# Attention, soft mixture and feed-forward in one kernel: ScalarE's order at the end of a round, and the second head's results in the other half of the partitions

## The reference

```python
def _attn_ref(r, k, v, w, u):            # B 4, H 8, S 768, D 48
    state = zeros(B, H, D, D)
    for t in range(S):
        kt, vt, rt, wt = k[:, :, t], v[:, :, t], r[:, :, t], w[:, :, t]
        cur = einsum('bhd,bhe->bhde', u[None] * kt, vt)
        y[:, :, t] = einsum('bhd,bhde->bhe', rt, state + cur)
        state = wt[..., None] * state + einsum('bhd,bhe->bhde', kt, vt)
    return y
# x = y as (B*S, H*D) = 3072 x 384, then
# _moe_ref: soft mixture with 8 experts of 4 slots, x @ phi, two softmaxes, relu MLPs of 1024
# _moe2_ref: h = relu(x @ w_in) (3072 x 2048); (h * h) @ w_out
```

## Time and profile before

| what | us |
|---|---|
| median of 3 runs | 537.76 |
| lowest and highest run | 533.3, 538.28 |
| the profiled execution | 541.06 |
| its span | 539.1 |
| of it, from the span's start to the end of attention's last copy | 252.1 |
| a round in the middle (level(rd, 0, 1) to the next) | 26.6 |

### The profile page before, as it was taken

One profiled execution on the slowest core, in us unless ns is written; L12 is line 12 of the kernel. 1 busy time (PEld: TensorE's weight loads), 2 busy tenths in 40 slices (PEclk: granted clock), 3 DMA queues, 4 the chain that ended last, 5 costly groups with the idle time before them and its releaser, 6 DMA issues.

```text
span 539.1 us, 18119 instructions
## 1 busy us (share of the span) xinstructions
PE 487.9 (91%) x7516; PEld 432.1 (80%) x7516; DVE 334.0 (62%) x583; ACT 333.9 (62%) x689; POOL 13.7 (3%) x21
## 2 busy tenths in 40 slices
PE   5688989798989898788889899999999999999996
PEld 3576878687878786777435489999999999999996
DVE  8687888788888787743441286555555555555552
ACT  5677786778787777453222376666566656665663
POOL 9000000000000000000000000000000000000000
PEclk9888999999999999979999999999999999999999
DMA  8785375757363614764999430101010101010101
GB/s 166 135 171 117 69 180 110 179 114 127 60 125 64 119 26 139 212 208 136 316 399 373 144 117 1 45 1 45 0 46 1 44 0 44 0 44 1 45 0 44
DMA packets 129385, 56.19 MB, mean 104 GB/s; under 512 B 103328, under 2 KB 128928, under 8 KB 128928
## 3 DMA queue, kind: packets, MB, share of 16 engines
q1 hardware_dynamic: 126112, 54.53, 38.6%
q10 hardware_dynamic: 3200, 0.59, 0.6%
HBM read 50.38 MB, written 4.72 MB: 102 GB/s over the span
## 4 chain that ended last, share of the span: by engine, by line
PE 71%; ACT 11%; SPq 6%; issue 5%; DVE 4%; DMA 2%; ACTq 0%; DVEq 0%
PE bank L758 13%; PE bank L760 12%; PE bank L759 12%; PE lbank L482 5%; ACT wide L855 5%; PE ybank L526 4%; PE bank L748 4%; PE ybank L542 4%; PE tbank L433 4%; SPq L282 3%; SPq L374 2%; PE lbank L509 2%; PE lbank L493 2%; DMA w_hi<-in_moe_w_dram 2%; ACT aa L865 1%
## 5 line engine op out<-in xcount | busy, mean ns | idle before, releaser
L758 PE MATMUL bank<-wo_high,h_high 128*128 128x384 f32 x384 | 128.8, 335 | 1.4 <-DVE h_low L1253 1.2
L759 PE MATMUL bank<-wo_low,h_high 128*128 128x384 f32 x384 | 128.4, 334 | 0.0
L760 PE MATMUL bank<-wo_high,h_low 128*128 128x384 f32 x384 | 128.4, 334 | 0.0
L999 ACT ACTIVATE h_relu<-bank 128x384 f32<-128x384 f32 x128 | 63.0, 492 | 72.7 <-PE bank L748 72.4
L1251 DVE CAST h_high<-h_sq 128x384 fp32r<-128x384 f32 x128 | 46.0, 359 | 95.1 <-PE bank L760 86.3
L1087 DVE TENSOR_TENSOR rk<-rk,wl 112x768 f32<-112x768 f32 x80 | 76.5, 956 | 40.6 <-PE lbank L482 22.4
L1253 DVE TENSOR_TENSOR h_low<-h_sq,h_high 128x384 fp32r<-128x384 f32 x128 | 71.5, 559 | 4.4
L758 PEld LDWEIGHTS bank<-wo_high,h_high 128*128 128x128 f32 x384 | 72.1, 188 | 2.6 <-issue 2.2
L759 PEld LDWEIGHTS bank<-wo_low,h_high 128*128 128x128 f32 x384 | 72.1, 188 | 0.0
L760 PEld LDWEIGHTS bank<-wo_high,h_low 128*128 128x128 f32 x384 | 72.1, 188 | 0.0
L1003 ACT ACTIVATE h_sq<-h_relu 128x384 f32<-128x384 f32 x128 | 67.4, 527 | 4.1
(11 more groups left out here) (127 smaller groups left out, 547.6 us busy)
## 6 DMA issues: line engine op xcount, KB each, us to landing
w_sb<-in_moe_w_dram SPq DMA_DIRECT2D x32, 384.0 KB, 4.1
w_hi<-in_moe_w_dram SPq DMA_DIRECT2D x16, 384.0 KB, 9.2
v_tok<-in_v_dram SPq DMA_DIRECT2D x32, 144.0 KB, 3.1
w_lo<-in_moe_w_dram SPq DMA_DIRECT2D x1, 4608.0 KB, 16.4
out_dram<-o_sb SPq DMA_DIRECT2D x8, 576.0 KB, 3.0
nat<-in_r_dram SPq DMA_DIRECT2D x62, 72.0 KB, 2.5
nat<-in_k_dram SPq DMA_DIRECT2D x62, 72.0 KB, 2.6
nat<-in_w_dram SPq DMA_DIRECT2D x60, 72.0 KB, 2.6
```

The costliest lines, as they stand in the source:

```text
L758: nc.tensor.matmul(acc, hi, wo_high[:, fb, :], start=(fb == 0), stop=False)
L759: nc.tensor.matmul(acc, hi, wo_low[:, fb, :], start=False, stop=False)
L760: last = nc.tensor.matmul(acc, lo, wo_high[:, fb, :], start=False, stop=(fb == NF - 1))
L999: nc.scalar.activation(h_relu[fb % 2][:], h_bank[fb % 2][:, 0:GT * P], ACT.Relu).then_inc(relu_done, 1)
```

## The change

It has two parts. First, ScalarE's order: at the end of a round it copies the second pair's top level (`top_level_out(rd, 1)`) ahead of widening the first pair for the next round, and the widening of the second pair (`widen(rd+1, 1, 1)`) moves into the next round, between the two `k_out`. Second, `y_near` and `y_far` write the results of head 1 to the other half of the partitions (`par ^ h` in place of `par`); `y_to_x` copies head 0's bank as before in one activation of 128 partitions, and head 1's bank in two activations of 64 partitions that swap the halves back. `y_evac` so counts three for each pair and round in place of two.

```diff
+    Y_OUT = 3
-                eng.wait_ge(y_evac[s], 2 * ROUNDS)
+                eng.wait_ge(y_evac[s], Y_OUT * ROUNDS)
...
+            def y_rows(par, h):
+                half = par ^ h
+                return slice(C * half, C * half + C)
+
             def y_near(rd, s):
...
                             rows = slice(C * par, C * par + C)
                             at = 512 * h + i * D
-                            last = nc.tensor.matmul(ybank[rows, at:at + D], aa[rd % 2][s][rows, PER * h + i, :],
+                            last = nc.tensor.matmul(ybank[y_rows(par, h), at:at + D], aa[rd % 2][s][rows, PER * h + i, :],
                                                     v_tok[s][rd % (1 + s)][rows, i, h, :], start=(i == 0), stop=False,
                                                     skip_group_check=True)
...
             def y_far(rd, s):
...
-                            rows = slice(C * par, C * par + C)
                             at = 512 * h + i * D
-                            last = nc.tensor.matmul(ybank[rows, at:at + D], rk[rd % 3][s][a:b, 0, C * c:C * c + C],
+                            last = nc.tensor.matmul(ybank[y_rows(par, h), at:at + D], rk[rd % 3][s][a:b, 0, C * c:C * c + C],
...
             def y_to_x(rd, s):
                 act.wait_ge(y_mm[s], rd + 1)
-                for h in range(2):
-                    src = ybank[:, 512 * h:512 * h + PER * D].rearrange("p (i n) -> p i n", n=D)
+                for h, a, b, to in ((0, 0, P, 0), (1, C, P, 0), (1, 0, C, C)):
+                    src = ybank[a:b, 512 * h:512 * h + PER * D].rearrange("p (i n) -> p i n", n=D)
                     at = s * PW + h * D
-                    nc.scalar.activation(X[:, :, rd, at:at + D], src, ACT.Copy).then_inc(y_evac[s], 1)
+                    nc.scalar.activation(X[to:to + b - a, :, rd, at:at + D], src, ACT.Copy).then_inc(y_evac[s], 1)
...
                 if late:
                     k_out(rd - 1, 0)
-                if late:
+                    widen(rd, 1, 1)
                     k_out(rd - 1, 1)
...
                 next_out(10, 2)
+                top_level_out(rd, 1)
                 if ahead:
                     widen(rd + 1, 0, 1)
-                top_level_out(rd, 1)
-                if ahead:
-                    widen(rd + 1, 1, 1)
```

More of the change, by code:

```diff
@@ L360, in _ @@
                 for s in range(2):
-                    sp.wait_ge(y_evac[s], 2 * ROUNDS)
+                    sp.wait_ge(y_evac[s], Y_OUT * ROUNDS)
                 sp.dma_start(debug, X[:].rearrange("p a b c -> p (a b c)")).then_inc(stored[0], 16)
@@ L455, in k_times_v @@
                 if s == 0 and rd > 0:
-                    pe.wait_ge(y_evac[1], 2 * rd)
+                    pe.wait_ge(y_evac[1], Y_OUT * rd)
                 if s == 1:
@@ L519, in y_near @@
                 else:
-                    pe.wait_ge(y_evac[0], 2 * (rd + 1))
+                    pe.wait_ge(y_evac[0], Y_OUT * (rd + 1))
                 for i in range(PER):
@@ L608, in _ @@
                 pe.wait_ge(top_out[s], 2 * ROUNDS)
-                pe.wait_ge(y_evac[s], 2 * (ROUNDS - 1))
+                pe.wait_ge(y_evac[s], Y_OUT * (ROUNDS - 1))
             turn_x(0, 4)
```

## The result

| | before | after |
|---|---|---|
| median of 20 runs, us | 536.35 | 533.33 |
| lowest and highest | 533.24, 541.4 | 530.86, 536.73 |
| profiled execution and its span | 541.06, 539.1 | 535.5, 533.7 |

The ratio is 0.995, with a 95% interval of 0.9928 to 0.9973: 2.7 us faster (3.0 by the medians), not the 14.7 that I had forecast, and less than the 1% that I called a difference. The time is 533.33 us; forecast were 523.1 and a range of 519 to 532.5.

The account below looks back on a forecast made before the run. A dependence loop hopping between TensorE and ScalarE was taken to bound the round. Savings of 1.2 + 11.4 + 1.06 + 1.08 = 14.7 us, off the median 537.76, gave 523.1 us, range 519 to 532.5.

Parts of the forecast that it names:

- The order: ScalarE's queue at a round's end: k_out of pair 0 no longer waits behind pair 1's widening, 1.16 us a round.
- The near matmuls: TensorE's y_near on four array quarters instead of two: 33.7 to 19.4 ns a matmul, 0.69 us less a block.
- B: Rival: y_near gains nothing because both row halves write into the same PSUM bank; 531.7 us, chance 0.14.
- C: Rival: y_near comes down only to y_far's pace, 0.30 us a block; 526.9 us, chance 0.13.
- D: Rival: slower, matmuls of y_near take turns at the banks; 557.6 us if one by one, chance 0.05.
- The third copy ... I take the same 0.30: ScalarE's y_to_x: one more activation costs 0.30 us, on the loop for pair 1.
- My upper bound of 1.1: Upper bound on the third copy's cost in y_to_x, 1.1 us, if each of the two took twice its time.
- The cover of pair 0's copy: Pair 0's y_to_x: the extra copy's 0.30 us is hidden; emptying ends by 142.9, TensorE's second turn begins at 143.0.
- Six rounds give 1.9 each, 11.4: Attention's six rounds each get 1.9 us shorter (1.16 + 0.69 + 0.37 - 0.30), 11.4 us together.
- above 25.5 with L526 at 19 ns: Sign against the prediction: rounds above 25.5 us though y_near reaches 19 ns, meaning a missed VectorE or ScalarE wait.
- The last round: Last round and tail: two y_near give 1.06 us, two more behind it less the last copy 1.08; forecast gain 2.1.
- E: Clock rival: two more stretches at the lower clock give 529.7 us, one fewer 520; chance of more 0.11.

Follow-up runs that it names:

- e11: Kernel before with ScalarE's new order alone and 24 of the 32 w1 loads moved behind attention; ratio 1.0202 against the kernel before.
- e9: Kernel before with 24 of the 32 w1 loads moved behind attention; ratio 1.0405 against the kernel before.
- e7: Changed kernel with its third copy beginning at partition 0 (64 partitions, into its own tile), head 1's halves left swapped; ratio 0.9892 against the kernel before.
- e4: Changed kernel with three copies of the same sizes, none crossing partitions, head 1's rows left swapped; ratio 0.9887 against the kernel before.
- e3: Changed kernel without the third copy: two copies of 128 partitions, head 1's rows left swapped; ratio 0.9808 against the kernel before.
- e2: Changed kernel with ScalarE's old order, so swapped halves and third copy alone; ratio 1.0084 against the kernel before, 4.5 us slower.
- e6: Changed kernel with the 12 w1 loads beside the last round moved behind attention; ratio 1.0146 against the kernel before.
- e14: Kernel before with ScalarE's new order alone, on one chip with the changed kernel; ratio 0.9882 against the kernel before, median 531.43 us.
- e13: Changed kernel with only two copies of 128 partitions and 24 w1 loads moved behind attention; ratio 1.0161 against the kernel before.
- e5: Kernel before with the 12 w1 loads beside the last round moved behind attention; ratio 1.0253 against the kernel before.
- e12: Changed kernel with head 1's two half copies in the other order, low half first; ratio 0.9889 against the kernel before.
- e8: Changed kernel with two ScalarE copies of 128 partitions and GpSimd swapping head 1's halves into X; ratio 0.99 against the kernel before.

## Why the prediction was wrong

- **The order**: right in place and size, 1.16 forecast, 1.15 in the trace of the changed kernel, 1.02 a round in e11 against e9.
- **The near matmuls**: right in themselves, 19.4 ns forecast, 20.6 measured; B, C and D are out. That the measured 533.33 lies nearest to B's 531.7 is chance: what B needed, L526 at 34 ns, did not occur. The page "TensorEngine Tiling (Array Packing)" of the Trainium skill speaks under "Restrictions and Gotchas", Gotcha 1, of row tiles that can't access one bank at the same time; with four quarters writing both banks, 20.6 ns a matmul doesn't bear it out.
- **"The third copy ... I take the same 0.30" is the first step that failed.** It costs 0.69 (1.29 for three, 0.60 for two). Half a tile's partitions are not what makes it dear (e7), nor is crossing (e4). Each copy begins 0.43 after the one ahead if it reads or writes from another first partition, else 0.30. The change takes that overlap from all three copies. The sign stood in the trace that I had: the two activations of `widen`, on partitions 0 and 64, last 533 ns each in the mean (the page's group of L855) and 1.04 to 1.14 together, with no overlap, beside 0.71 for the two of 408. My upper bound of 1.1 held it; the chosen value came from the wrong row.
- **The cover of pair 0's copy** failed with it: 0.69 us and not 0.30 had to fit into a slack of some 0.45 (the input copy of before ends at 142.55, TensorE wants its tile at 143.0), and 0.39 came through. Together with pair 1 this makes the loop gain 1.0 a round in place of 1.9: over 5 us in six rounds, and 0.56 in the tail. With the copy's measured price the walk gives a round of 25.63 us for the change, 24.84 for e7, 24.54 for e3, 25.49 for the order alone and 26.78 for e2; the shortest rounds without a stop are 25.63 (in e6; 25.80 in the changed kernel itself), 24.84, 24.56, 25.57 (e14) and 26.75.
- **"Six rounds give 1.9 each, 11.4" is the second.** The rounds of the changed kernel are 25.8 to 27.45 us, "above 25.5 with L526 at 19 ns", and the wait that I missed is none of VectorE's or ScalarE's but TensorE's for nothing named. The trace of before has four stops of 1 us (ending at 104.65, 185.52, 214.31 and 228.64), and the sum took them as constant without saying so. They are 5.8 us in the trace of before and 9.5 in that of after. e13 shows the effect best: a shorter block whose gain hardly arrives, with a stop in every round. And e7 bounds it: a kernel that does pay 0.30 for its third copy gains 5.8 us, not 14.7, so more of the miss lies here and in the last round than in the copy.
- **The last round**, forecast at -2.1, came out at +2.8, with stops of 4.95 us in place of 2.57, 0.56 for the last copies and one more stretch at the lower clock. e5 and e6 show that the loads beside it are what makes the difference: with w1 elsewhere both kernels take 41.4 and 41.3 us there. That is still not the gain of 2.1. The clock was a rival (E); over the whole execution the lower level did not become more frequent.

That these stops are TensorE's own instructions arriving late is an inference, but the traces bear it out. They fall at the same places of the program before and after, and they shrink when data loads are moved away (e5, e6, e9). The page of the changed kernel lists, on queue q8, 58 packets of kind "instruction" with 0.95 MB in all, 16 KB each, and the traces keep the time of each. In all 17 traces a given packet starts at nearly the same matmul of TensorE's program, whatever the time is by then: the 24th behind 2970 to 2975 of the 7516 matmuls, the 31st behind 3876 to 3919. They land 4.6 to 5.0 us apart in the mean. And every one of the 164 stops in these traces ends 1.06 to 1.69 us after such a packet has landed; that of 2.40 us ends at 222.98, behind the packet that lands at 221.51.

The Trainium skill, "Runtime: NRT & Kernel Launch", "Instruction fetch mechanics", says that each engine's instructions are refilled in blocks of 16 KiB by a DMA queue of its own, and that the cost is mostly hidden. The size agrees with the queue's row; hidden it was not, with a stop of 2.40 us.

Two things stay open. Why the packets come late: they take 1.1 us each in the mean with w1's loads beside them and without, so what delays them should lie before their start. And the arithmetic: in e13 waits over 0.15 us make up 0.6 us a round, of 0.9 that are missing.

## What to carry to other kernels

Before a copy is added to a queue, look in the trace for a pair that already begins on another partition than its neighbour: whether it overlaps its neighbour is a third of its price (0.30 and 0.43 us here), and a copy put between two others can take the overlap from them as well. When a block of TensorE's is made shorter, read the "issue" waits first and see if they stand at fixed places in its program; here they took such a gain back, and beside heavy loads more than it. An "issue" behind which a semaphore stands in the code is another thing: look there before you count it. To check a walk along a loop, compare it with the rounds that have no stop; to forecast the time, add what the others lose. A two-part change should be timed in its parts: here one part gave 1.2 to 1.6% and the other lost half of it or more.

## What the hardware showed that I had not expected

- ScalarE: copies of 288 columns follow each other in 0.30 us if both read from the same first partition and write from the same one, with 64 or 128 of them (e7), and in 0.43 us if either differs (e4, e12); each lasts 0.41.
- TensorE: mid-program stops of up to 2.4 us with no semaphore, at the same matmul before and after, each ending 1.1 to 1.7 us after a 16 KB packet of the instruction queue has landed; 4.95 us of them in the last round beside w1's loads and 1.5 without (e6).
- GpSimd's copy of 64 x 288 takes 0.55 us, and VectorE's updates, as a mean of 80, 985 ns for 956 in a kernel that has 32 of them (e8).
